# Means from rounded operands, another chain for the last batch, other fold, bank and low-split orders in an attention, gated FFN, Fourier mixing and MLP kernel

## The reference

```
scores = q k^T / 8;  drop scores below max - tau;  p = exp(scores - max)
a = p / (sum(p) + 1e-09) @ v                       # per batch and head -> x (576 x 512)
xk, xr = mu * x + (1 - mu) * x shifted by one row
v2 = relu(xk @ w_k)^2 @ w_v;   x2 = sigmoid(xr @ w_r) * v2
u = x2 + real(fft over channels of (fft over rows of x2))
un = (u - mean(u)) / sqrt(var(u) + 1e-06)          # over the 512 channels
out = u + relu(un @ w_ch1) @ w_ch2
```

## Time and profile before

| | |
|---|---|
| median of 3 runs | 1093.48 us |
| profiled execution, its own time | 1093.62 us |
| its span (first to last instruction) | 1091.8 us |
| granted clock of PE, mean | 0.997 |
| busy: PE, DVE, ACT, POOL | 1057.1, 570.7, 511.4, 400.6 us |
| attention and dense stages, about | 0 to 681 us |
| MLP | 681 to 1092 us |

### The profile page before, as it was taken

How to read it: one execution, slowest core, us unless ns; L and a number is a source line. 1 busy time by engine, 2 the same in 40 slices (tenths; PEclk the granted TensorE clock), 3 DMA queues, 4 the chain that set the end, 5 groups by cost and what they waited for, 6 DMA issues and landing times.

```text
span 1091.8 us, 18457 instructions
## 1 busy us (share of the span) xinstructions
PE 1057.1 (97%) x7088; PEld 1000.6 (92%) x7088; DVE 570.7 (52%) x1096; ACT 511.4 (47%) x1250; POOL 400.6 (37%) x347
## 2 busy tenths in 40 slices
PE   6999999999999999999999889999999999999998
PEld 6899999998999999999999888888888888888998
DVE  7998765466865566864465755443123223223211
ACT  5988875646875746875656632221111111111110
POOL 5897664423663433563413534331111111111000
PEclk9999999999999999999999989999999999999999
DMA  8634202033302032301123108300200200200000
GB/s 240 186 110 168 57 25 57 3 110 90 101 25 58 18 118 67 101 24 35 45 67 109 44 1 301 122 1 1 70 1 1 70 1 1 69 1 1 36 1 34
DMA packets 43800, 70.10 MB, mean 64 GB/s; under 512 B 4288, under 2 KB 25664, under 8 KB 43200
## 3 DMA queue, kind: packets, MB, share of 16 engines
q1 hardware_dynamic: 43408, 68.59, 20.1%
q10 hardware_dynamic: 304, 0.33, 0.1%
HBM read 56.50 MB, written 12.41 MB: 63 GB/s over the span
## 4 chain that ended last, share of the span: by engine, by line
PE 80%; DVE 10%; ACT 4%; issue 3%; POOL 2%; DMA 0%; SPq 0%; DVEq 0%; ACTq 0%; POOLq 0%
PE PB L780 20%; PE PB L782 20%; PE PB L781 20%; PE PB L840 9%; PE PB L807 6%; PE PB L823 5%; DVE probs L1343 4%; DVE neg_s L1332 2%; ACT mix_v L1145 1%; ACT exps L1074 1%; DVE rowinv L1353 1%; DVE mix_v L1362 1%; ACT mix_h L1160 1%; POOL fold_l L703 1%; DVE k_sq L1432 1%
## 5 line engine op out<-in xcount | busy, mean ns | idle before, releaser
L1288 ACT ACTIVATE h_hi<-PB 128x464 fp32r<-128x464 f32 (+1 forms) x80 | 44.4, 555 | 335.5 <-PE PB L782 335.5
L1530 DVE SCALAR_TENSOR_TENSOR h_lo<-PB,h_hi 128x464 fp32r<-128x464 f32 (+1 forms) x80 | 51.0, 637 | 260.7 <-ACT h_hi L1288 260.7
L840 PE MATMUL PB<-v_sb,probsT 128*128 128x64 f32 (+1 forms) x1440 | 177.5, 270 | 0.0
L840 PEld LDWEIGHTS PB<-v_sb,probsT 128*128 128x128 f32 x1440 | 172.1, 192 | 0.0
L1343 DVE SCALAR_TENSOR_TENSOR probs<-neg_s,thresh,exps 128x576 f32<-128x576 f32 x144 | 156.2, 1084 | 0.2 <-issue 0.2
L1332 DVE TENSOR_SCALAR_CACHE_REDUCE neg_s<-PB,taus 128x576 f32<-128x576 f32 x144 | 117.0, 812 | 47.9 <-PE PB L807 43.7
L1083 ACT ACTIVATE probsT<-PB 128x384 f32<-128x384 f32 (+1 forms) x288 | 109.4, 433 | 68.6 <-PE PB L823 66.8
L780 PE MATMUL PB<-un_h,w1h 128*128 128x464 f32 (+1 forms) x320 | 121.6, 380 | 0.0
L782 PE MATMUL PB<-un_h,w1l 128*128 128x464 f32 (+1 forms) x320 | 118.9, 371 | 0.0
L781 PE MATMUL PB<-h_lo,w2h 128*128 128x464 f32 (+1 forms) x320 | 118.9, 371 | 0.0
L780 PE MATMUL PB<-h_hi,w2h 128*128 128x464 f32 (+1 forms) x320 | 118.8, 371 | 0.0
(11 more groups left out here) (174 smaller groups left out, 2341.2 us busy)
## 6 DMA issues: line engine op xcount, KB each, us to landing
q_raw<-qT_dram SPq DMA_DIRECT2D x62, 160.0 KB, 3.2
k_raw<-kT_dram SPq DMA_DIRECT2D x64, 144.0 KB, 3.1
w_raw<-w_dram SPq DMA_DIRECT2D x8, 1024.0 KB, 9.3
cs<-cs_scr SPq DMA_DIRECT2D x8, 870.0 KB, 6.8
u_scr<-x2T SPq DMA_DIRECT2D x4, 1152.0 KB, 4.8
cd<-cd_scr SPq DMA_DIRECT2D x4, 1032.0 KB, 4.9
v_sb<-v_dram SPq DMA_DIRECT2D x16, 256.0 KB, 2.9
u_in<-u_scr SPq DMA_DIRECT2D x4, 928.0 KB, 5.7
```

The source lines that it names most:

```text
L840: last = nc.tensor.matmul(bank(6 + p)[:, i * DH:i * DH + width], probsT[:, n % 2, kt * P128:(kt + 1) * P128], v_sb[:, kt, pair % 2, p * DH ...
L1530: nc.vector.scalar_tensor_tensor(h_lo[:, ft % 3, 0:w], bank(4 + ft % 3)[:, 0:w], 0.0, h_hi[:, ft % 3, 0:w].bitcast(F32), ALU.max, ALU.subt ...
```

## The change

It has nine parts. (1) `rowsum` gets a second column that holds epsilon, and the addition becomes a sum over the pair. (2) The tau operations stand behind the first head's splits in DVE's order. (3) The lows of w_k are made in eight half pieces at other tiles; table and w_v lows go one by one. (4) In a fold, the sum is folded before the difference is made. (5) The ring of four banks begins at 0, and the wait for all maxima moves from the u stage of the batch before last to the first transposes of the last batch. (6) The sums for means are split into high and low on POOL, and a mean is two fp32r matmuls. (7) Mixing steps 10 to 14 of the last batch come up to one slot earlier. (8) The chain of chunk 0 stands elsewhere: sum after mixing low 11, mean after r1, centring and square at v0, variance, root and Newton steps one v0 group later, the rounding of the result after the fifth k1 tile. (9) The split of the first w2 quarter goes behind the last y.

```diff
-MIX_AT_ALONE = [3, 4, 6, 7, 8, 9, 10, 11, 13, 14, 15, 16, 18, 18, 19, 19]
+MIX_AT_ALONE = [3, 4, 6, 7, 8, 9, 10, 11, 13, 14, 14, 15, 17, 18, 18, 19]
+WK_LOW_AT = {17: ((0, 0),), 21: ((0, 1),), 22: ((1, 0),), 25: ((1, 1),), 31: ((2, 0),), 32: ((2, 1),), 34: ((3, 0),), 35: ((3, 1),)}
-    two, four, six = [... for banks in ((2, 3), (2, 3, 0, 1), (6, 5, 0, 1, 2, 3))]
+    two, four, six = [... for banks in ((2, 3), (0, 1, 2, 3), (6, 5, 0, 1, 2, 3))]
-        rowsum = m.put("rowsum", [P128, TILES_PAIR], F32)
+        rowsum = m.put("rowsum", [P128, TILES_PAIR, 2], F32)
         part = r.put("part", [P128, 2, W], F32)
+        part_l, part_h = low.put("part_l", [P128, W], F32R), low.put("part_h", [P128, W], F32R)   # same place as part
# POOL
-                nc.gpsimd.memset(rowsum[:, :], 1.0).then_inc(pool_ready, 1)
+                nc.gpsimd.memset(rowsum[:, :, :], EPS_SM).then_inc(pool_ready, 1)
-                    if n == 17:
-                        wk_low(0)
-                        wk_low(1)
-                    if n in (21, 22):
-                        wk_low(n - 19)
-                    if n == 26:
-                        cd_low(0)
-                        cd_low(1)
-                    if n == 30:
-                        cs_low(0)
-                        cs_low(1)
-                    if n == 31:
-                        cs_low(2)
-                    if n in (35, 39, 40, 44):
-                        t = {35: 0, 39: 2, 40: 4, 44: 6}[n]
-                        wv_low(t)
-                        wv_low(t + 1)
+                    if n in WK_LOW_AT:
+                        for t, half in WK_LOW_AT[n]:
+                            wk_low(t, half)
+                    if n in (26, 27):
+                        cd_low(n - 26)
+                    if 28 <= n < 28 + ST:
+                        cs_low(n - 28)
+                    if n in (36, 37, 42, 43, 44, 45, 46, 47):
+                        wv_low(n - 36 if n < 38 else n - 40)
                         if stage == "k" and c == 0 and alone(d):
-                            yield 14
+                            yield mix_at(d, 11) + 1
 ...
                     nc.gpsimd.tensor_tensor(part[:, 0, 0:w], part[:, 0, 0:w], part[:, 1, 0:w], ALU.add).then_inc(done, 1)
+                    pool.wait_ge(done, c * 4 + 2)
+                    rounded(part_h[:, 0:w], part[:, 0, 0:w]).then_inc(done, 1)
+                    pool.wait_ge(done, c * 4 + 3)
+                    nc.gpsimd.tensor_tensor(part_l[:, 0:w], part[:, 0, 0:w], part_h[:, 0:w].bitcast(F32), ALU.subtract).then_inc(done, 1)
# PE
+                def over_channels(c):
+                    w = width_of(c)
+                    nc.tensor.matmul(mean_out(c), mean512[:, :].bitcast(F32R), part_h[:, 0:w], start=True, stop=False)
+                    return nc.tensor.matmul(mean_out(c), mean512[:, :].bitcast(F32R), part_l[:, 0:w], start=False, stop=True)
-                    nc.tensor.matmul(mean_out(c), mean512[:, :], part[:, 0, 0:width_of(c)], start=True, stop=True).then_inc(mean_ready, 1)
+                    over_channels(c).then_inc(mean_ready, 1)
+                        if dt == 0 and alone(d):
+                            pe.wait_ge(max_ready, TILES)
+                                if alone(d) and c == 1 and i == 3:      # r
+                                    mean(0)
-                                if alone(d) and c == 0 and i == 5:      # k
-                                    mean(0)
-                                if alone(d) and c == 0 and i == 1:      # v
+                                if alone(d) and c == 0 and i == 2:
                                     variance(0)
-                        if g == 0 and drains(d):
-                            pe.wait_ge(max_ready, TILES)
# ACT
-                                if alone(d) and c == 1 and dt == 1:     # r
-                                    square(0)
-                                if alone(d) and c == 1 and ft == 2:     # k
+                                if alone(d) and c == 1 and ft == 4:
                                     norm_hi(0, 0)
-                                yield slot_of(d, "v", 0, 1, 1)
+                                yield slot_of(d, "v", 0, 0)
+                                square(0)
+                                yield slot_of(d, "v", 0, 2, 1)
                                 root(0)
# DVE (the four tau operations now stand behind the first head's k_lo)
-                        nc.vector.tensor_scalar(rowinv[:, tiles], rowsum[:, tiles], EPS_SM, None, ALU.add).then_inc(sum_ready, 1)
+                        nc.vector.tensor_reduce(rowinv[:, tiles], rowsum[:, tiles, :], axis=AX.X, op=ALU.add).then_inc(sum_ready, 1)
-                                if alone(d) and c == 0 and ft == KFT - 1:   # k
-                                    center(0, 0)
                                 yield slot_of(d, "v", 0, 0)
-                                split_w2(0, True)
-                                split_w2(0, False)
+                                center(0, 0)
-                                    if i == 1:
+                                    if i == 2:
                                         var_eps(0)
                                         inverse_root(0)
                                         newton(0)
+                    if alone(d):                                        # behind the last y
+                        split_w2(0, True)
+                        split_w2(0, False)
 ...
                     nc.vector.tensor_tensor(pair_sum[:, :], x2T[:, t, :], x2T[:, 3 - t, :], ALU.add).then_inc(pair_ready, 1)
-                    nc.vector.tensor_tensor(pair_dif[:, :], x2T[:, t, :], x2T[:, 3 - t, :], ALU.subtract).then_inc(pair_ready, 1)
                     nc.vector.memset(fold_v[:, t, 1, ends], 0.0)
-                    dve.wait_ge(pair_ready, d * 4 + t * 2 + 2)
+                    dve.wait_ge(pair_ready, d * 4 + t * 2 + 1)
                     nc.vector.tensor_copy(fold_v[:, t, 0, ends], pair_sum[:, ends])
                     nc.vector.tensor_tensor(fold_v[:, t, 0, near], pair_sum[:, near], pair_sum[:, far], ALU.add).then_inc(fold_ready, 1)
+                    nc.vector.tensor_tensor(pair_dif[:, :], x2T[:, t, :], x2T[:, 3 - t, :], ALU.subtract).then_inc(pair_ready, 1)
+                    dve.wait_ge(pair_ready, d * 4 + t * 2 + 2)
                     nc.vector.tensor_tensor(fold_v[:, t, 1, near], pair_dif[:, near], pair_dif[:, far], ALU.subtract).then_inc(fold_ready, 1)
```

More of the change, by code:

```diff
@@ L179, in bank_turns @@
     of, before, had = {}, {}, {}
-    two, four, six = [itertools.cycle(banks) for banks in ((2, 3), (2, 3, 0, 1), (6, 5, 0, 1, 2, 3))]
+    two, four, six = [itertools.cycle(banks) for banks in ((2, 3), (0, 1, 2, 3), (6, 5, 0, 1, 2, 3))]
     for group in order:
@@ L366, in build @@
         assert early.at <= r.at
+        at = r.at
         part = r.put("part", [P128, 2, W], F32)
+        low = Place(at)
+        part_l, part_h = low.put("part_l", [P128, W], F32R), low.put("part_h", [P128, W], F32R)
+        assert low.at == r.at
         un_h, un_l, sqr, row_stats = [], [], [], []
@@ L842, in pv @@
                     last.then_inc(pv_ready, 1)
+                def over_channels(c):
+                    w = width_of(c)
+                    nc.tensor.matmul(mean_out(c), mean512[:, :].bitcast(F32R), part_h[:, 0:w], start=True, stop=False)
+                    return nc.tensor.matmul(mean_out(c), mean512[:, :].bitcast(F32R), part_l[:, 0:w], start=False, stop=True)
                 def mean(c):
-                    pe.wait_ge(sums, c * 2 + 2)
+                    pe.wait_ge(sums, c * 4 + 4)
                     if c > 0:
                         pe.wait_ge(vare_ready, c)
-                    nc.tensor.matmul(mean_out(c), mean512[:, :], part[:, 0, 0:width_of(c)], start=True, stop=True).then_inc(mean_ready, 1)
+                    over_channels(c).then_inc(mean_ready, 1)
                 def variance(c):
-                    pe.wait_ge(sq_sums, c * 2 + 2)
+                    pe.wait_ge(sq_sums, c * 4 + 4)
                     pe.wait_ge(cent_ready, c + 1)
-                    nc.tensor.matmul(mean_out(c), mean512[:, :], part[:, 0, 0:width_of(c)], start=True, stop=True).then_inc(var_ready, 1)
+                    over_channels(c).then_inc(var_ready, 1)
                 def wait_evicted(*group):
@@ L1263, in _ @@
                 act.wait_ge(pool_ready, 1)
-                nc.scalar.activation(exps[:, 0, 0:1], rowsum[:, 0:1], ACT.Exp)
+                nc.scalar.activation(exps[:, 0, 0:1], rowsum[:, 0, 0:1], ACT.Exp)
                 act.wait_ge(qk_in[0], 64)
@@ L1344, in mask @@
                                                    exps[:, n % 2, :], ALU.is_le, ALU.mult,
[L1345 removed]
+                                                   accum_out=rowsum[:, jj, 0:1]).then_inc(probs_ready, 1)
                     if jj in (TAIL, TILES_PAIR - 1):
```

20 lines of the change are left out of this document (10 added, 10 removed).

## The result

The changed kernel takes 1088.31 us (median of 5; 1086.84 to 1088.97) against 1093.48 before: ratio 0.9948 [0.9937, 0.9960]. It is faster by 5.2 us, where 12.9 were forecast, and lies 0.8 us outside the range. The profiled execution took 1086.97 us, span 1085.2, so 6.6 us of span have to be found in the trace (this execution is one of the two fastest of the five).

What follows compares the result with a forecast made beforehand. TensorE, busy for 97% of the span, was taken as the bound, so gains come from its waits, slow stretches or less work. Seven terms summed to 12.9 us: 1093.6 - 12.9 = 1080.7 us, range 1073.5 to 1087.5.

Steps and rivals of the forecast that it cites:

- rival (b): Last batch: variance chain so late that the clock falls all the same, 8.3 us lost instead of 4.0; 1085.0 us, 12%.
- rival (d): Tiles 26 to 48: POOL sets the pace, a head's splits ending over two tiles later; slower, 1096.3 us, 5%.
- opening: Start: tau operations leave the head of DVE's queue, first scores come sooner; gain 0.3 us (0 to 0.6).
- epsilon, pieces, lows: First stage: short reduction and half pieces give 3.5 us back up to tile 39, lateness takes 1.0; gain 2.5 us.
- folds: Folds: first fold ready about 0.7 us earlier, but later operations may wait for POOL; taken as 0 (-1.2 to 2.0).
- drain banks: First transposes of the last batch: the 0.92 us wait for the eviction goes; gain 0.9 us (0 to 0.9).
- mean of chunk 0: Mean moved behind the second r stage: matmul 0.35 us shorter, same kind of wait; gain 0.4 us (-2 to 1.6).
- variance of chunk 0: Last batch: loss falls from 10.0 to 4.0 us, a 3.6 us wait without a clock fall; gain 6.0 us.
- other means: Other chunks' means: two rounded matmuls cost 0.42 us instead of 0.77, extra POOL work hidden; gain 2.8 us.
- The forecast's own sign of falling: Last batch: the prediction falls if it doesn't get shorter by at least 3 us.
- the sign of being right: First stage: scores from tile 11 to 39 in 66 us would show the prediction right.
- rival (c): First stage: the reduction waits for POOL like the addition and nothing is gained there; 1083.2 us, 7%.

Runs made afterwards that it cites:

- e5: The kernel before with only the epsilon addition replaced by the reduction over pairs; 1091.01 us, ratio 0.9973.
- e1: The changed kernel with the eight value-weight lows back at their old tiles, two whole tiles each; 1085.09 us, ratio 0.9920.
- e7: e1 with the key weights' and tables' lows also back at their old tiles and sizes; 1083.01 us, ratio 0.9896.
- e3: The changed kernel with the fold order undone, sums and differences taken first again; 1087.16 us, ratio 0.9943.
- e6: The changed kernel with the last batch's variance product alone taken in full precision from the unrounded sum; 1085.76 us, ratio 0.9925.
- e2: The changed kernel with the last batch's variance product and its inverse root one group of products later; 1084.03 us, ratio 0.9916.
- e8: e1 with the variance product one group later and the chain behind it spread out over later groups; 1081.27 us, ratio 0.9882.
- e4: The changed kernel with the reduction undone, epsilon added by the scalar addition again; 1088.44 us, ratio 0.9955.
- e9: The kernel before with the rounded means alone, every place kept; 1093.98 us, ratio 1.0000.
- e11: The changed kernel with means and variances in full precision again, last stage in its new order; 1085.14 us, ratio 0.9921.
- e10: The changed kernel with old low places and fold order, variance and its chain later, first MLP weights rounded behind the fold; 1078.46 us, ratio 0.9861.
- e12: e10 with VectorE's opening in the old order, tau operations ahead of the first key rounding; 1077.06 us, ratio 0.9846.

## Why the prediction was wrong

The last batch went as rival (b) has it, the clock falling after a wait shorter than the 5.4 us that it names, and the first stage as a mild form of rival (d), with GpSimd's work in the way. Term by term, in us of the two profiled executions:

| step | forecast | measured | what decided |
|---|---|---|---|
| opening | 0.3 | -0.15 | lead at tile 9 |
| epsilon, pieces, lows | 2.5 | -1.45 | tiles 9 to 48: 2.48 for the reduction (e5), -2.09 for the pieces (e1 against e7), -1.84 for the value lows (the change against e1) |
| folds | 0 | -0.3 | tiles 48 to 143; 0.2 of it by e3 |
| drain banks | 0.9 | 1.1 | the wait of 0.92 in the earlier trace rows is gone |
| mean of chunk 0 | 0.4 | 1.5 | the wait of 0.80 at 613.39 is gone, the product is cheaper; its own wait 0.45 instead of 0.49 |
| variance of chunk 0 | 6.0 | 3.0 | wait 4.1, forecast 3.6; the clock fell |
| other means | 2.8 | 2.9 | 408.05 against 410.9 |
| sum | 12.9 | 6.6 | |

Of the 6.3 us that are missing, 4.4 lie in the first stage and 3.0 in the variance; the other terms came out 1.1 better together, most of it by the wait of 0.80 us that went, for which the forecast has no term; that is luck. The forecast's own sign of falling, a last batch that gets less than 3 us shorter, did not come (4.5 us shorter): it watched the stage that missed by less.

**Variance: "too short for the clock to fall, which took some 5 us".** This step failed; rival (b), at 12%, had it. The wait itself was forecast well (3.6 against 4.11), and so was what was lost before (10.0; 22.87 - 12.8 = 10.07). But one fall of the clock was taken for the rule: 5 us in the earlier trace rows, 2.3 us in the changed kernel, after the end of a wait of 2.2 us in e6, after a wait of 1.21 us none at all. What remains lost is 19.84 - 12.8 = 7.0 us, not 4.0: the wait of 4.1, the pair's 0.4, and 2.5 us for the work from 631.84 to 636.9 at a granted clock of 0.50, which is the price that rival (b) put on it. e2 and e8 got 5.4 of the 7.0 back by placing the product where hardly anything waits (0.96 and 0.95 us).

**Pieces and value lows: "I give 3.5 back up to tile 39 and take 1.0 for lateness after it".** This is the other step that failed, and the larger one: both sizes were wrong, and the second reverses the sign of the whole term. Scores from tile 11 to tile 39 take 67.90 us, where 66 would have been the sign of being right (69.57 before), so 1.7 us came back and not 3.5. Then 3.1 us were lost up to tile 48, not 1.0. Without the pieces the reduction gives 2.57 us up to tile 39 and keeps all but 0.1 of it (e5, e7): the two moves of lows cost what the reduction gains, and 1.45 us more.

The prediction named this cost (GpSimd has "little idle time to catch up in") and put it at 5% as rival (d), asking for more than two tiles of lateness. It does not take that: masks and mixing operations run beside any low that is moved out of idle time. And GpSimd did have idle time, 4.88 us ahead of its first mixing low in the trace of before; the change moved four lows from before that gap to behind it. That gap was not looked for. (The bound of 8.7 us for eight additions comes to 8.6, which changes nothing.) By medians the value lows cost 3.3 us and the pieces 2.9; these differences carry the scatter of the first tiles as well.

**The reduction** was right in its row (0.2 forecast, 0.165 measured) and rival (c) false, but its worth depends on the rest: 2.7 us alone, nothing that the times tell in the changed kernel (e4). The Trainium skill, page "VectorE: DVE Perf Modes", section "Rules for kernel authors", calls the tensor reduction the slowest operation and warns of it on a hot path; for ten elements to a partition the trace differs: 0.167 us at most, where the scalar addition took 0.171 at least and up to 1.40. The Trainium skill, page "SBUF — State Buffer", section "SBUF: two separate sides", has ports that VectorE and GpSimd share and that one of them holds to its instruction's end, VectorE when it reads two SBUF operands or runs in a two-port mode; the mask of 1.98 us, which reads two, and a reduction that reads one and never waits agree with it.

**Rounded means: "the two operations more on POOL ... are hidden".** True of the eight products in the MLP, where 2.9 us came out for the 2.8. For chunk 0 the lengthening was in the chain (five operations were counted), but its price was not set against the gain. e9 and e11 show it: 2.9 us won in the MLP, 3.0 lost in the last batch of the kernel before and 4.7 in that of the changed one. In e10 and e12 the variance no longer waits for the low part, their MLP takes 408.05 and 408.0 us and their last batch 81.25 and 81.33, so the gain seems to be kept there; no run takes the rounding out of these two.

**Folds, drain banks, sum.** The second fold did wait for GpSimd (0.93 us for 0.45 at 571.13 in the changed kernel), the first low came sooner, and zero was a fair forecast (-0.2 by e3). The drain banks gave what the row said.

## What to carry to other kernels

Before moving work of an engine that blocks a neighbour, find its idle stretches and see whether the work lies in one now; spreading it evenly can be worse than a burst just ahead of idle time. A wait of the matmul engine is priced with the clock that follows it, and a product behind a long chain belongs where its operands are surely there, with the chain behind it cut into bits that fit between the consumer's operations. A cheaper format that lengthens the chain ahead of it is worth its saving only where nobody waits for that chain. And compare traces by stretches: a lead carries everything that an execution met before.

## What the runs showed of the hardware that was not expected

The granted clock does not fall after a fixed idle time. Waits of 4.0 to 4.1 us at one and the same product stand in the changed kernel, e1, e3, e4 and e7, and the clock fell 2.3, 4.4, 2.6, 1.9 and 3.5 us after PE fell idle (in e1 that is after the wait had ended). Elsewhere it fell 5.1 us into a wait in the kernel before, 5.2 at e9's variance, 1.9 in e5, 2.3 at e9's mean, and in e6 only after a wait of 2.2 us had ended. Single waits of 0.95, 0.96 and 1.21 us in the last batch of e8, e2 and e11 left it at 1.00, and so did waits of 1.19 and 1.56 us in the first stage of the changed kernel; but in e6 the clock fell 0.4 us after the same two, in e8 1.2 us after one of 1.15, and in e2 several short gaps in four microseconds were followed by 0.58. Once down it stayed at 0.50 for 3.4 to 10.2 us (e2, e5).

Executions of the same first stage end between 0.84 and 3.49 us behind. They part in the first nine tiles, by up to 1.9 us, and two things are seen there. In e6 (as in e10) PE keeps its slow pace, 0.24 us from one score product to the next, up to 15.6 us; in e3 it is at 0.13 from 14.2 on. And in the changed kernel, whose pace is up as early as e3's, the masks of 15.44 and 17.63 take 1.31 and 1.95 us beside GpSimd, the same two in e3 0.81 and 0.95. What makes an execution go one way or the other is open.
